# Own buffers for two more q and k pairs, two score and mask buffers in chunk 0, and v scaled by ScalarE there

## What is computed

```python
# 1: linear attention with decay, 8 heads of 64
for t in range(S):
    state = gamma * state + einsum('bhd,bhe->bhde', k[:, :, t], v[:, :, t])
    y[:, :, t] = scale * einsum('bhd,bhde->bhe', q[:, :, t], state)
# 2: x is [3072, 512], w_in [512, 2048], w_out [2048, 512]
h = x @ w_in
x = (maximum(h, 0) + alpha * minimum(h, 0)) @ w_out
# 3: one of 8 experts per token, by cosine to expert_emb over tau
out[mask] = gate_w[mask] * (maximum(x[mask] @ w1[e], 0) @ w2[e])
```

## Time and profile before

| | us |
|---|---|
| median of 3 runs (lowest, highest) | 1031.23 (1031.12, 1033.36) |
| profiled execution | 1031.7 |
| its span | 1030.0 |
| TensorE busy with matmuls | 962.7 (93%) |
| VectorE, ScalarE, GpSimd busy | 580.1, 253.3, 248.0 |

### The profile page before, as it was taken

The page is one execution under the profiler, slowest core; times in us unless marked ns, Lnnn a source line. Parts: engine busy times, 40 slices in busy tenths (PEclk is TensorE's granted clock), DMA queues, the critical chain, the costliest instruction groups (busy, mean ns, idle before and its releaser), DMA issues.

```text
span 1030.0 us, 16630 instructions
## 1 busy us (share of the span) xinstructions
PE 962.7 (93%) x5422; PEld 794.1 (77%) x5423; DVE 580.1 (56%) x1057; ACT 253.3 (25%) x396; POOL 248.0 (24%) x200
## 2 busy tenths in 40 slices
PE   3999999999999999999999999459999999999994
PEld 3777778887888788878887888348888888888883
DVE  3554569745974598459834973853273332523540
ACT  2222111112111111111102110423353332523541
POOL 5152223331433143313341223410011000100000
PEclk9899999999999999999999999769999999999998
DMA  7333250015001400140011031175155241433310
GB/s 247 117 131 113 83 165 1 1 42 164 0 0 41 163 0 0 41 143 1 1 42 52 1 149 55 62 270 202 41 184 211 68 172 41 138 121 121 120 42 30
DMA packets 26302, 92.01 MB, mean 89 GB/s; under 512 B 3951, under 2 KB 4079, under 8 KB 21888
## 3 DMA queue, kind: packets, MB, share of 16 engines
q1 hardware_dynamic: 17872, 70.37, 19.1%
q0 software_dynamic: 4432, 13.40, 3.4%
q10 hardware_dynamic: 3952, 7.63, 2.7%
HBM read 78.77 MB, written 15.78 MB: 92 GB/s over the span
## 4 chain that ended last, share of the span: by engine, by line
PE 82%; DVE 5%; issue 4%; DMA 4%; POOL 2%; ACT 1%; SPq 0%; ACTq 0%; POOLq 0%; DVEq 0%
PE bank L596 22%; PE bank L605 22%; PE bank L688 15%; PE bank L712 14%; DMA attention<-in_qk 3%; PE bank L699 2%; PE bank L508 2%; PE bank L524 1%; PE bank L547 1%; PE bank L672 1%; DVE scratch L800 1%; DVE scratch L805 1%; DVE en_all L983 1%; ACT activations_split L1122 1%; POOL activations_split L1315 1%
## 5 line engine op out<-in xcount | busy, mean ns | idle before, releaser
L605 PE MATMUL bank<-weights_split,activations_split 128*128 128x512 f32 x1152 | 278.9, 391 | 6.9 <-POOL activations_split L1315 3.9
L596 PE MATMUL bank<-activations_split,weights_split 128*128 128x512 f32 x1152 | 279.0, 392 | 0.0
L605 PEld LDWEIGHTS bank<-weights_split,activations_split 128*128 128x128 f32 x1152 | 215.0, 188 | 57.7 <-DVE activations_split L811 5.9
L596 PEld LDWEIGHTS bank<-activations_split,weights_split 128*128 128x128 f32 x1152 | 216.2, 189 | 45.9 <-issue 1.2
L1315 POOL TENSOR_TENSOR activations_split<-scratch,activations_split 128x512 fp32r<-128x512 f32 x84 | 114.7, 1366 | 338.7 <-ACT activations_split L1122 331.4
L1122 ACT CAST activations_split<-scratch 128x512 fp32r<-128x512 f32 x96 | 59.8, 623 | 430.3 <-DVE scratch L805 430.3
L688 PE MATMUL bank<-weights_split,activations_split 128*128 x648 | 156.9, 398 | 2.5 <-DVE activations_split L1030 2.5
L712 PE MATMUL bank<-weights_split,activations_split 128*128 x648 | 154.5, 394 | 2.3 <-DVE activations_split L1061 2.3
L688 PEld LDWEIGHTS bank<-weights_split,activations_split 128*128 128x128 f32 x648 | 121.8, 191 | 27.4 <-issue 3.1
L712 PEld LDWEIGHTS bank<-weights_split,activations_split 128*128 128x128 f32 x648 | 119.7, 188 | 26.4 <-issue 2.5
L865 DVE SCALAR_TENSOR_TENSOR attention<-rows,en_all 128x512 f32<-128x512 f32 x140 | 135.0, 1005 | 0.0
(11 more groups left out here) (138 smaller groups left out, 667.4 us busy)
## 6 DMA issues: line engine op xcount, KB each, us to landing
attention<-in_w_exp SPq DMA_DIRECT2D x24, 1024.0 KB, 5.1
attention<-in_qk SPq DMA_DIRECT2D x24, 512.0 KB, 3.9
attention<-in_kv SPq DMA_DIRECT2D x43, 256.0 KB, 3.7
en_all<-in_w_exp SPq DMA_DIRECT2D x8, 1024.0 KB, 7.1
rows<-in_w_mlp SPq DMA_DIRECT2D x14, 512.0 KB, 3.2
rows<-expert_rows ACTq DMA_DIRECT2D x27, 257.0 KB, 3.0
en_all<-en_rows SPq DMA_DIRECT2D x1, 1792.0 KB, 7.0
expert_rows<-in_pad_rows SPq DMA_DIRECT2D x4, 257.0 KB, 4.6
```

Source lines behind the costliest of these rows:

```text
L596: last = mm(H_ps[f % 2][:, :], win(a, kc, f), x[:, kc, :], start=(k == 0), stop=(k == 3 * KC - 1))
L605: last = mm(bank[j][:, :], x[f % 2][:, j * P:(j + 1) * P], wout(a, f), start=(f == 0 and n == 0), stop=(f == FB - 1 and n == 2))
```

## The change

- **q and k buffers.** Pairs 0 and 1 keep their buffers. Pairs 2 and 3 get their own: in chunk 0 inside `en_all` (`qk_first`), from chunk 1 on inside `scratch` (`qk_late`), where the feed-forward part has `neg` and `g_sb`. So no q/k load of chunk 0 waits. In chunk c the loads of pairs 2 and 3 wait for the last low part of chunk c - 1 (`s_gl`) and are issued one behind the other; loads of pairs 0 and 1 of the next chunk are issued in the turns of pairs 0 and 1. GpSimd scales queries 2 and 3, then v 3.
- **The broadcast.** Before it fills `en_all`, SP also waits for `s_en_last`, since `qk_late` covers the embeddings and is loaded behind it.
- **Chunk 0's attention.** A second pair of score banks (6 and 7) and a second mask buffer (in `en_all`). TensorE makes scores of a pair ahead of the values of the one before. v is scaled by ScalarE, two halves a pair, and GpSimd scales only q. The splits of weight blocks 0 to 2 move in the lists of ScalarE and VectorE.
- **The state copies.** In chunk 0's feed-forward part VectorE copies a state one block later than TensorE makes it.

```diff
     def by_batch(x):
...
-    qk_sb = [part(2 * TB) for _ in range(2)]
-    qT, kT = ([by_batch(x[:, i * TB:(i + 1) * TB]) for x in qk_sb] for i in range(2))
+    qk_slot = [part(2 * TB) for _ in range(2)]
...
+    qk_first = [EN[:, (1 + 2 * i) * TB:(3 + 2 * i) * TB] for i in range(2)]
+    Am_first = [Am, EN[:, 5 * TB:7 * TB].rearrange("p (h b c) -> p h b c", h=2, b=B)]
...
+    def qk_sb(c, hp):
+        late = qk_first if isinstance(c, int) and c == 0 else qk_late
+        return qk_slot[hp] if hp < 2 else late[hp - 2]
+    def qT(c, hp):
+        return by_batch(qk_sb(c, hp)[:, 0:TB])
+    def kT(c, hp):
+        return by_batch(qk_sb(c, hp)[:, TB:2 * TB])
...
+    qk_late = [Y[:, 2 * i * TB:2 * (i + 1) * TB] for i in range(2)]
...
+    A0_ps = [[A_ps[:, 0], A_ps[:, 1]], [b3(6), b3(7)]]
...
-    s_qk_ld = [sem(f"qk_ld{i}") for i in range(2)]
+    s_qk_ld = [sem(f"qk_ld{i}") for i in range(HP)]
+    s_vs_first = sem("vs_first")
...
             def load_qk(c, hp):
-                u = 4 * c + hp
-                if isinstance(u, int) and 2 <= u < 6:
-                    sp.wait_ge(s_A, due(s_A, u - 1))
-                elif not (isinstance(u, int) and u < 2):
-                    sp.wait_ge(s_Yi, due(s_Yi, u - 5))
+                first = isinstance(c, int) and c == 0
+                if not first and hp >= 2:
+                    sp.wait_ge(s_gl, due(s_gl, FB * c))
+                elif not first and isinstance(c, int) and c == 1:
+                    sp.wait_ge(s_A, due(s_A, hp + 1))
+                elif not first:
+                    sp.wait_ge(s_Yi, due(s_Yi, 4 * c + hp - 7))
...
-                sp.dma_start(qk_sb[hp % 2], qk[bass.ds(c, 1), hp].rearrange("o p n -> p (o n)"))\
-                  .then_inc(s_qk_ld[hp % 2], 16)
+                sp.dma_start(qk_sb(c, hp), qk[bass.ds(c, 1), hp].rearrange("o p n -> p (o n)"))\
+                  .then_inc(s_qk_ld[hp], 16)
...
+            sp.wait_ge(s_en_last, due(s_en_last, 1))
...
                 for hp in range(HP):
-                    if hp < 2:
-                        load_qk(c, hp + 2)
-                    elif following:
-                        load_qk(c + 1, hp - 2)
...
+                        load_qk(c, 2)
+                        load_qk(c, 3)
...
-                    elif following:
-                        load_v(c + 1, hp % 3)
...
+                    if hp and following:
+                        load_v(c + 1, hp % 3)
+                    if hp < 2 and following:
+                        load_qk(c + 1, hp)
...
             def scores(c, hp):
...
+                first = isinstance(c, int) and c == 0
...
-                if not (isinstance(u, int) and u == 0):
+                if not first:
...
-                if hp == 0 and not (isinstance(c, int) and c == 0):
+                elif hp >= 2:
+                    pe.wait_ge(s_m, due(s_m, u - 1))
+                if hp == 0 and not first:
...
+                dst = A0_ps[hp % 2 if first else 0]
...
                     for hh in range(2):
...
-                        last = mm(A_ps[:, hh, b, :], kT[hp % 2][rows, b, :], qT[hp % 2][rows, b, :],
+                        last = mm(dst[hh][:, b, :], kT(c, hp)[rows, b, :], qT(c, hp)[rows, b, :],
...
                     for hh in range(2):
...
-                        last = mm(Y_ps[hp % 2][rows, b, :], St[rows, hp, b, :], qT[hp % 2][rows, b, :],
+                        last = mm(Y_ps[hp % 2][rows, b, :], St[rows, hp, b, :], qT(c, hp)[rows, b, :],
...
+            def scaled(c, hp):
+                if isinstance(c, int) and c == 0:
+                    pe.wait_ge(s_vs_first, due(s_vs_first, hp + 1))
+                else:
+                    pe.wait_ge(s_vs, due(s_vs, 4 * (c - 1) + hp + 1))
             def to_state(c, hp, dst):
...
-                pe.wait_ge(s_vs, due(s_vs, u + 1))
+                scaled(c, hp)
...
             def values(c, hp, first=False):
...
-                pe.wait_ge(s_vs, due(s_vs, u + 1))
+                scaled(c, hp)
+                mixed = Am_first[hp % 2] if first else Am
...
                     for hh in range(2):
...
-                        last = mm(Y_ps[hp % 2][cols, b, :], v_sb(c, hp)[:, b, cols], Am[:, hh, b, :],
+                        last = mm(Y_ps[hp % 2][cols, b, :], v_sb(c, hp)[:, b, cols], mixed[:, hh, b, :],
...
+            scores(0, 0)
             for hp in range(HP):
-                scores(0, hp)
+                if hp + 1 < HP:
+                    scores(0, hp + 1)
...
-            def attention(c, first=False, extra=None):
+            def masked(c, hp, src, dst):
+                for hh in range(2):
+                    ins = ve.scalar_tensor_tensor(dst[:, hh], src[hh], chunk_growth(2 * hp + hh),
+                                                  causal.unsqueeze(1).broadcast_to([P, B, P]), ALU.mult, ALU.mult)
+                ins.then_inc(s_m, 1)
+            def attention(c):
                 for hp in range(HP):
...
-                    if not (first and hp == 0):
-                        dve.wait_ge(s_Y, due(s_Y, u))
-                    for hh in range(2):
-                        ins = ve.scalar_tensor_tensor(Am[:, hh], A_ps[:, hh], chunk_growth(2 * hp + hh),
-                                                      causal.unsqueeze(1).broadcast_to([P, B, P]), ALU.mult, ALU.mult)
-                    ins.then_inc(s_m, 1)
+                    dve.wait_ge(s_Y, due(s_Y, u))
+                    masked(c, hp, A0_ps[0], Am)
...
-                    if extra is not None:
-                        extra(hp, 0)
-                    if not first and not is_last(c):
+                    if not is_last(c):
...
+            def first_attention():
+                for hp in range(HP):
+                    dve.wait_ge(s_A, due(s_A, hp + 1))
+                    if hp >= 2:
+                        dve.wait_ge(s_Y, due(s_Y, hp - 1))
+                    masked(0, hp, A0_ps[hp % 2], Am_first[hp % 2])
+                    if hp:
+                        x_low(0, hp - 1)
+                    if hp == 1 or hp == 3:
+                        split_w(hp // 2)
+                x_low(0, HP - 1)
+                split_w(2)
...
-                    if isinstance(c, int) and c == 0 and f in SU_AT:
-                        hp = SU_AT[f]
+                    if isinstance(c, int) and c == 0 and f - 1 in SU_AT:
+                        hp = SU_AT[f - 1]
...
-            attention(0, first=True, extra=lambda hp, when: split_w(hp - 1) if when == 0 and hp > 0 else None)
+            first_attention()
...
-            def attention(c, extra=None):
+            def x_high(c, hp):
+                act.wait_ge(s_Y, due(s_Y, 4 * c + hp + 1))
+                se.copy(x_hi[:, hp, :].rearrange("p (b c) -> p b c", b=B), Y_ps[hp % 2]).then_inc(s_xh, 1)
+            def attention(c):
                 for hp in range(HP):
-                    u = 4 * c + hp
-                    if extra is not None:
-                        extra(hp, 0)
-                    if extra is not None:
-                        extra(hp, 1)
-                    act.wait_ge(s_Y, due(s_Y, u + 1))
-                    se.copy(x_hi[:, hp, :].rearrange("p (b c) -> p b c", b=B), Y_ps[hp % 2]).then_inc(s_xh, 1)
+                    x_high(c, hp)
+            def first_values(hp):
+                ld = s_v_first if v_sb(0, hp) is v_first else s_v_ld[hp % 3]
+                act.wait_ge(ld, due(ld, 16))
+                for hh in range(2):
+                    v4 = v_sb(0, hp)[:, :, hh * D:(hh + 1) * D]
+                    ins = se.activation(v4, v4, ACT.Copy, scale=vdecay[:, 2 * hp + hh:2 * hp + hh + 1])
+                ins.then_inc(s_vs_first, 1)
...
-            attention(0, extra=lambda hp, when: split_w(hp) if when == 1 and hp < AHEAD else None)
+            act.wait_ge(s_masks, due(s_masks, 16))
+            first_values(0)
+            first_values(1)
+            x_high(0, 0)
+            split_w(0)
+            first_values(2)
+            x_high(0, 1)
+            first_values(3)
+            x_high(0, 2)
+            split_w(1)
+            x_high(0, 3)
+            split_w(2)
...
             def value_decay(c, hp):
-                u = 4 * c + hp
-                if v_sb(c, hp) is v_first:
-                    pool.wait_ge(s_v_first, due(s_v_first, 16))
-                else:
-                    pool.wait_ge(s_v_ld[hp % 3], due(s_v_ld[hp % 3], 16 * (2 * c + hp // 3 if hp % 3 == 0 else c + 1)
-                                                     if not (isinstance(c, int) and c == 0) else 16))
+                pool.wait_ge(s_v_ld[hp % 3], due(s_v_ld[hp % 3], 16 * (2 * c + hp // 3 if hp % 3 == 0 else c + 1)))
...
             def query_decay(c, hp):
-                pool.wait_ge(s_qk_ld[hp % 2], due(s_qk_ld[hp % 2], 16 * (2 * c + hp // 2 + 1)))
+                pool.wait_ge(s_qk_ld[hp], due(s_qk_ld[hp], 16 * (c + 1)))
...
-                gp.tensor_tensor(qT[hp % 2], qT[hp % 2], qdecay[:, hp:hp + 1, :].broadcast_to([P, B, P]), ALU.mult)\
```

(4 more changed lines are left out.)

## The result

| | before | changed |
|---|---|---|
| median, us | 1031.55 | 1018.88 (1017.32 to 1019.87) |
| profiled execution, us | 1031.7 | 1019.52 |
| its span, us | 1030.0 | 1017.9 |

The ratio is 0.9873 with a 95% interval of 0.9854 to 0.9891: 12.7 us faster. The forecast was 1016.1, in a range of 1013.4 to 1020.2, so the range holds the time and the point lies 2.8 us under it. Lines are those of the changed kernel now: scores L530, values L576, to_state L563, hidden L625, down L634, masks L807, state copy L864, query scaling L1354, last embedding matmul L674, q/k loads L384, broadcast L452. A row at the end of a window counts only the instructions that start inside it.

The account below looks back on a forecast made before the run. The prediction took TensorE as the bound (82% of the chain), winnable only where it stands still or runs at its lower clock. Terms -7.6 - 5.6 + 1.6 - 3.5 = -15.1 gave 1016.1 us, range 1013.4 to 1020.2.

Parts of the forecast that it names:

- Part 1: Chunk 0's attention: early q/k loads and the new order start the feed-forward part sooner; gain 7.6 us, bounds 5 to 9.
- the walk: Chunk 0's attention: new order stepped through with profiled durations, putting the hidden layer's start at 21.6 us, not 27.93.
- Part 2: Chunk 0's feed-forward: state copies one block later remove four TensorE stops, 1.41 us each; gain 5.6 us, bounds 3.8 and 6.0.
- Part 3: Chunk 1: the later broadcast delays the third pair's load; stall 3.0 us, net loss 1.6 us.
- (a): Rival: the clock falls in chunk 1's new gap, costing 2.6 and up to 3.3 us: 1018.9; chance 0.20.
- Part 4: Chunks 2 to 5: q/k loads of pairs 2 and 3 issued before the attention remove waits; gain 3.5 us (3.2 to 4.2).
- (c): Rival: VectorE falls behind elsewhere, so chunk 0's four state-copy stops remain in another block: 1021.7; chance 0.04.
- (d): Rival: slower than before, as the broadcast holds SP's queue in chunk 1: 1032 to 1034; chance 0.02.
- (b): Rival: chunk 0 gives about 2.6 us less, through a clock fall or ScalarE's longer list: 1018.7; chance 0.12.

Follow-up runs that it names:

- E5: Changed kernel with chunk 0's attention in the old order and buffers, v scaled by GpSimd, only the early q/k loads kept there; 1022.39 us.
- E4: Changed kernel with chunk 0's v scaled by GpSimd again and ScalarE's v steps left out; 1018.99 us.
- E10: Kernel before the change with only chunk 0's state copies moved one block later; 1025.20 us.
- E2: Changed kernel with chunk 0's state copies back in the block in which TensorE makes the state; 1023.16 us.
- E1: Changed kernel with SP's wait for the last embedding matmul moved behind broadcast and pad rows, ahead of the first late q/k load; 1013.07 us, again 1012.82.
- E3: Changed kernel with three extra 512-column matmuls on TensorE ahead of the scores of chunk 1's third pair; 1016.87 us.
- E9: E7 with the loads of the next chunk's pairs 0 and 1 back in the turns of pairs 2 and 3; 1020.89 us.
- E11: E9 with SP's list in the chunks exactly as before the change, also the waits of pairs 0 and 1 and v ahead of k; 1020.03 us.
- E8: E1 with five extra 256-column matmuls on TensorE before the first scores, results unused; 1012.94 us.
- E7: E1 with q/k loads of pairs 2 and 3 in chunks 1 to 5 issued behind from_state again, own buffers kept; 1028.20 us.

## Why the prediction was right, and where it was off

| step | forecast, us | profiled execution, us |
|---|---|---|
| 1, chunk 0 to down 1 | -7.6 | -8.8 |
| 2, state copies | -5.6 | -5.0 |
| 3, chunk 1 | +1.6 | +5.0 |
| 4, chunks 2 to 5 | -3.5 | -3.7 |
| rest of the span | 0 | +0.4 |
| sum | -15.1 | -12.1 |

**Part 1** held in its order: the walk had hidden at 21.6, and it was 20.57. Scores 0 began 0.24 us earlier and values 0 ended 0.5 us earlier, which VectorE's list passed on; the third pair's mask (16.41) came 0.7 us before my 17.1. The clock stayed up over the two gaps (24 matmuls of hidden in 5.73 us). The loads carry somewhat over half of it (E5), the second buffers the rest, v on ScalarE nothing that shows (E4); the prediction had not split it so. The forecast and the 8.8 both count from a trace in which the clock had fallen ahead of hidden; against E10's, where it had not, the step is 7.2 us (39.31 to 32.14).

**Part 2** was over-sized by 0.15 us a stop: 17.17 us for the group, where I had 17.01: the 12 hidden matmuls behind to_state take 2.94 us in the chain, not 2.72. E2 and E10 show the mechanism.

**Part 3** is the step that failed: a loss of 1.6 us was forecast and 5.0 measured. Its queue was right: the stall was 3.43 us by the profile, 3.0 forecast, and the load landed at 123.0, which on the old scale is 136.8, the upper end given. E1 shows that the place of that one wait makes it. What was wrong was to price the step without the clock. The rival (a) had the price, 2.6 to 3.3 us, and the runs 2.8 (6.43 less 3.60); it had a chance of 0.20, and occurred in all five profiled executions that had the gap. The row I read for it, a fall within a 4.39 us gap, bore more on a 3 us gap than I gave it. 1016.1 + 2.8 is 1018.9. The page "TensorE: Matmul & The Clock Gate" of the Trainium skill says in "What's actually happening" that activity releases a throttle that is otherwise on. The trace agrees: the clock is 0.50 behind the gap, and 1.00 in E3, where TensorE was kept busy.

The page "DMA: Bandwidth & Descriptors" of the Trainium skill ("Queues, rings and completion order") has each DMA engine take descriptors in ring order. The third pair's load behind the broadcast did wait: it landed 7.5 us after its issue, against 3.1 in E1. E9 beside E11 hints at the other side: with the next loads sent close behind the fourth pair's, chunks 2 to 5 took 4.9 us more (422.0 against 417.1, 1.6 of it the clock), while chunk 1 went the other way. The prediction had costed at nothing a transfer issued behind a load that is waited for; these runs do not settle its price.

**Part 4** was right in size, and E11 shows the cause. The rivals (c) and (d) did not occur; (b) was the other way. Three of four steps were within 1.2 us. That the total is only 2.8 us off is in part luck: part 3 was 3.4 us too low, and 1.2 too little gain in part 1 made up for some of it.

## What to carry to other kernels

When a wait is added ahead of a large transfer, price the gap it makes twice: its length, and the clock behind it. Do not take a gap as safe by its length: here the clock fell behind one of 2.07 us and held behind one of 2.82. Before a buffer is moved into space that is read late, see which wait its user really needs: here the place of one wait cost 5.8 us beside a gain of 12.7, and E1, at 1013 us, beats both kernels. Issue a load that is on the path well before its use. Whether loads that nobody waits for should be kept from going out close behind it is worth a run of its own; here chunks 2 to 4 of E9 speak for it and chunk 1 does not.

## What the runs showed that I had not expected

- The clock fell behind gaps of 2.36 us (E8, after 1.24 us of work) and 2.07 us (E9, chunk 4), and held behind 2.31 (E9, chunk 2), 2.46 and 2.82 us (E7, chunks 2 and 3). In the kernel before it rose in the second scores and held over gaps of 1.4 us; in E10, the same code up to there, it stayed low over such gaps until about 25 us.
- At the start of every kernel the granted clock reads 1.00 while the matmuls have the lower clock's durations (16 scores 2.08 us at 7.3, against 1.16; in E8 the extra matmuls of 256 columns, 0.46 us each, as long as 0.47 for E3's of 512). In E10 that lasts to about 25 us. The duration is the better witness there.
- The first scores started between 6.5 and 7.8 us in the profiled executions, with the same loads ahead of them (the first pair's q and k landed at different times).
